# A spatial product made of seven block products, with all of v before all of u

## The reference

```
h = max(x @ w_in, 0)                      # x: 2 x 768 x 512, w_in: 512 x 1024
u, v = h[..., :512], h[..., 512:]
v_n = (v - mean(v)) / sqrt(var(v) + 1e-6) # over the 512 channels of a token
v_s = einsum('ts,bsd->btd', w_spatial, v_n) + b_spatial[None, :, None]   # w_spatial: 768 x 768
out = (u * v_s) @ w_out                   # w_out: 512 x 512
```

## Time and profile before

| | us |
|---|---|
| median of 3 runs | 501.73 |
| the profiled execution, its own time | 501.73 |
| its span (first to last instruction) | 499.9 |
| TensorE busy with matmuls | 494.2 |
| VectorE, ScalarE, GpSimd busy | 285.3, 214.9, 209.1 |

### The profile page before, as it was taken

The page is one execution under the profiler, slowest core; times in us unless marked ns, Lnnn a source line. Parts: engine busy times, 40 slices in busy tenths (PEclk is TensorE's granted clock), DMA queues, the critical chain, the costliest instruction groups (busy, mean ns, idle before and its releaser), DMA issues.

```text
span 499.9 us, 7893 instructions
## 1 busy us (share of the span) xinstructions
PE 494.2 (99%) x2822; PEld 414.2 (83%) x2822; DVE 285.3 (57%) x666; ACT 214.9 (43%) x502; POOL 209.1 (42%) x178
## 2 busy tenths in 40 slices
PE   8999999999999999999999999999999999999997
PEld 7788677887888888888888888888888998889985
DVE  5888788421379457455574654658686356521530
ACT  7988889532235533232341231324655113321121
POOL 6797576443346765762766616514330000000000
PEclk9999999999999999999999999999999999999999
DMA  8824501132223322202222022021400000110002
GB/s 235 267 89 116 182 2 44 45 126 85 84 86 101 110 84 86 82 2 85 85 85 84 1 84 74 20 88 63 147 1 1 1 1 21 43 64 0 1 24 103
DMA packets 14553, 36.29 MB, mean 73 GB/s; under 512 B 2480, under 2 KB 2480, under 8 KB 14512
## 3 DMA queue, kind: packets, MB, share of 16 engines
q1 hardware_dynamic: 12640, 32.35, 19.4%
q10 hardware_dynamic: 1872, 3.41, 1.8%
HBM read 32.61 MB, written 3.15 MB: 72 GB/s over the span
## 4 chain that ended last, share of the span: by engine, by line
PE 96%; ACT 3%; DMA 1%; issue 0%; SPq 0%; ACTq 0%
PE bank L1228 23%; PE bank L1502 15%; PE bank L1434 9%; PE bank L1359 9%; PE bank L1531 9%; PE bank L1524 9%; PE bank L1564 7%; PE bank L1284 4%; PE bank L1266 4%; PE bank L1251 3%; ACT prob L955 1%; PE bank L1298 1%; PE bank L1306 1%; DMA qk_raw<-in_qk 1%; PE bank L1331 1%; PE bank L1320 1%
## 5 line engine op out<-in xcount | busy, mean ns | idle before, releaser
L470 POOL TENSOR_TENSOR w_slot<-stage,w_slot 128x1024 fp32r<-128x1024 f32 x30 | 73.4, 2456 | 64.9 <-ACT w_slot L1025 64.8
L787 DVE TENSOR_TENSOR uT<-bank,uT 128x512 f32<-128x512 f32 x68 | 45.8, 690 | 25.1 <-PE bank L1531 23.1
L1228 PE MATMUL bank<-sp_slot,vn 128*128 128x384 f32 x288 | 50.3, 334 | 0.0
L1228 PEld LDWEIGHTS bank<-sp_slot,vn 128*128 128x128 f32 x288 | 50.0, 188 | 0.2
L955 ACT ACTIVATE prob<-prob,row_min 128x256 f32<-128x256 f32 (+1 forms) x96 | 45.9, 480 | 7.4 <-DVE row_min L605 7.4
L1502 PE MATMUL bank<-u_op,s_slot 128*128 128x512 f32 x192 | 47.6, 389 | 0.0
L1434 PE MATMUL bank<-hid,w_slot 128*128 128x512 f32 x192 | 46.9, 393 | 0.0
L1359 PE MATMUL bank<-u_split,w_slot 128*128 128x512 f32 x192 | 46.5, 391 | 0.0
L1524 PE MATMUL bank<-hid,w_slot 128*128 128x512 f32 x192 | 46.1, 389 | 0.0
L1531 PE MATMUL bank<-hid,w_slot 128*128 128x512 f32 x192 | 46.1, 389 | 0.0
L1434 PEld LDWEIGHTS bank<-hid,w_slot 128*128 128x128 f32 x192 | 35.7, 188 | 8.2 <-issue 0.9
(11 more groups left out here) (121 smaller groups left out, 837.5 us busy)
## 6 DMA issues: line engine op xcount, KB each, us to landing
stage<-in_w_ch SPq DMA_DIRECT2D x32, 512.0 KB, 3.3
qk_raw<-in_qk SPq DMA_DIRECT2D x23, 256.0 KB, 4.9
v_all<-in_v SPq DMA_DIRECT2D x12, 256.0 KB, 5.3
out_dram<-o_stage ACTq DMA_DIRECT2D x12, 256.0 KB, 2.0
stage<-in_w_spT SPq DMA_DIRECT2D x6, 384.0 KB, 3.0
stage<-in_w_in SPq DMA_DIRECT2D x4, 512.0 KB, 4.2
stage<-in_w_out SPq DMA_DIRECT2D x2, 512.0 KB, 3.6
V_raw<-in_V SPq DMA_DIRECT2D x4, 96.0 KB, 4.6
```

Source lines behind the costliest of these rows:

```text
L470: nc.gpsimd.tensor_tensor(dst[:, LO, :], stage[n % 2][:, 0:w], dst[:, HI, :].bitcast(F32), ALU.subtract).then_inc(w_lo, 1)
L787: vec.tensor_tensor(y, y_bank(e)[:], y, ALU.add).then_inc(y_sum, 1)
L1228: last = mm(out_ap, lhs(a), rhs(c), start=(n == 0), stop=(n == 3 * len(terms) - 1))
```

## The change

The spatial matrix product is cut into 2 x 2 x 2 blocks and made with 7 block products instead of 8, a Strassen-like scheme (the table `SEVEN`, which the pairs already use). The contracted tokens are halved into even and odd tiles, the output tokens into 384 and 384, the channels of two fb into 128 and 128. One group `("s", q)` stands for a batch and a pair of fb (q = 0 to 3); it makes the seven products x = 0 to 6 into four banks, each product 9 matmuls of 384 columns (3 tiles by 3 passes).

- Left operands: of each group three blocks of v (`v_one`) and four sums of blocks (`v_sum`), all split into high and low parts. Groups 0 and 1 (batch 0) do this with instructions of 384 columns, groups 2 and 3 (batch 1) with three times as many of 128 columns for the sums and for the single blocks. The four sums' low parts are four instructions of 384 columns. Group 2's low parts are made by GpSimd, the others by VectorE.
- Right operands: of the spatial weights seven blocks, four of them sums (`sum_sp`, `split_sp_sums`, on GpSimd, as is `split_sp`, the low part of the plain blocks).
- Outputs: the products are added up on VectorE (`add_bank`, `add_bias`, seven per group), with the bias of the first half of tokens; the second half gets it through `add_far` on GpSimd, which adds the difference of the two halves' biases.
- `ITEMS` is now: 12 v, 12 u, s 0, s 1, s 2, o 0 to 2, s 3, o 3 to 11. v tiles have 12 buffers of their own instead of 3.
- `LOADS` and the staging of the spatial weights: `in` 3 comes before the spatial loads, and a spatial load also waits for the sums of the pair before it. ScalarE rounds the last block of `y_split` after the spatial tiles 2 and 3, and takes no v tile before all of `y_split` is done.

The diff, cut to what the prediction speaks of:

```diff
--- before.py
+++ after.py
         LOADS = ([("w", m) for m in range(FT + 8)] + [("in", 0), ("in", 1)]
-                 + [("w", m) for m in range(FT + 8, 2 * FT)] + [("in", 2), ("sp", 0), ("sp", 5), ("in", 3)]
-                 + [("sp", s) for s in range(1, 5)] + [("out", 0), ("out", 1)])
+                 + [("w", m) for m in range(FT + 8, 2 * FT)] + [("in", 2), ("in", 3)]
+                 + [("sp", s) for s in range(NT)] + [("out", 0), ("out", 1)])
...
-        ITEMS = ([("v", 0), ("u", 0, 0), ("v", 1), ("u", 0, 1), ("v", 2), ("u", 0, 2), ("v", 3), ("u", 0, 3),
-                  ("v", 4), ("u", 1, 0), ("v", 5), ("u", 1, 1), ("u", 1, 2), ("u", 1, 3)]
-                 + [("s", 0, c, fb) for c in range(2) for fb in range(FB)]
-                 + [("v", 6), ("v", 7), ("o", 0), ("v", 8), ("o", 1), ("v", 9), ("o", 2), ("v", 10), ("o", 3),
-                    ("v", 11), ("o", 4), ("u", 2, 0), ("o", 5), ("u", 2, 1), ("u", 2, 2), ("u", 2, 3)]
-                 + [("s", 1, c, fb) for c in range(2) for fb in range(FB)] + [("o", t) for t in range(NT, TILES)])
+        ITEMS = ([("v", t) for t in range(TILES)] + [("u", c, fb) for c in range(CH) for fb in range(FB)]
+                 + [("s", 0), ("s", 1), ("s", 2), ("o", 0), ("o", 1), ("o", 2), ("s", 3)]
+                 + [("o", t) for t in range(3, TILES)])
+        V_DONE = TILES
...
+        def made(*what):
+            return sum(7 if w[0] == "s" else 1 for w in ITEMS[:item_no(*what) + 1])
+        def s_banks(q):
+            return g_ring[4:8] if q == 1 else g_ring[0:4]
+        GPART = (2, 1, 2, 3)
...
+            def add_far(q):
+                pool.wait_ge(b_diff, 1)
+                pool.wait_ge(g_dve, 7 * q + 2)
+                if q:
+                    pool.wait_ge(gate_lo, 4 * q)
+                nc.gpsimd.tensor_tensor(gpart[3][:], gpart[0][:], b_row[:, HT:S], ALU.add).then_inc(far_bias, 1)
...
+            for s in range(NT):
+                n = load_no("sp", s)
+                split_sp(s, n)
+                if s % 2:
+                    sum_sp(s // 2, n)
+                    split_sp_sums(s // 2)
+            split_v_sums(2)
+            add_far(0)
+            split_v_ones(2)
+            add_far(1)
+            split_out(load_no("out", 0))
+            split_out(load_no("out", 1))
+            add_far(2)
+            add_far(3)
...
+            def sum_v(q):
+                parts = v_blocks(q)
+                dve.wait_ge(vn_ok, NT * (q // 2 + 1))
+                if q < 2:
+                    dve.wait_ge(g_ps, made("u", q, FB - 1))
+                elif q == 2:
+                    for n in range(2):
+                        dve.wait_ge(v_one_hi[n], 3)
+                        dve.wait_ge(v_one_lo[n], 3)
+                else:
+                    dve.wait_ge(g_ps, made("s", 1))
+                def dst(name, ks):
+                    return v_sum_raw[V_BUF[q]][:, SUMS[name], ks, :]
+                for ks in parts:
+                    vec.tensor_tensor(dst("S1", ks), v_block(q, 1, 0, ks), v_block(q, 1, 1, ks),
+                                      ALU.add).then_inc(v_summed[q], 1)
+                for ks in parts:
+                    vec.tensor_tensor(dst("S3", ks), v_block(q, 0, 0, ks), v_block(q, 1, 0, ks),
+                                      ALU.subtract).then_inc(v_summed[q], 1)
+                dve.wait_ge(v_summed[q], len(parts))
+                for ks in parts:
+                    vec.tensor_tensor(dst("S2", ks), dst("S1", ks), v_block(q, 0, 0, ks),
+                                      ALU.subtract).then_inc(v_summed[q], 1)
+                dve.wait_ge(v_summed[q], 3 * len(parts))
+                for ks in parts:
+                    vec.tensor_tensor(dst("S4", ks), v_block(q, 0, 1, ks), dst("S2", ks),
...
+            def split_v_ones(q):
+                x = 0
+                for ks in v_blocks(q):
+                    for n, (r, half) in enumerate(ONES):
+                        x += 1
+                        dve.wait_ge(v_one_hi[q], x)
+                        hi, lo = v_one[V_BUF[q]][n]
+                        vec.tensor_tensor(lo[:, ks, :], v_block(q, r, half, ks), hi[:, ks, :].bitcast(F32),
+                                          ALU.subtract).then_inc(v_one_lo[q], 1)
+            def split_v_sums(q):
+                dve.wait_ge(v_sum_hi[q], 1)
+                for x in range(4):
+                    vec.tensor_tensor(v_sum[V_BUF[q]][:, LO, x, :, :], v_sum_raw[V_BUF[q]][:, x, :, :],
+                                      v_sum[V_BUF[q]][:, HI, x, :, :].bitcast(F32),
+                                      ALU.subtract).then_inc(v_sum_lo[q], 1)
...
+            def add_bank(q, dst, src, held, products, after):
+                dve.wait_ge(g_ps, made("s", q) - 7 + products)
+                if after:
+                    dve.wait_ge(g_dve, 7 * q + after)
+                vec.tensor_tensor(gpart[dst][:], gpart[src][:], s_banks(q)[held][:, 0:HT], ALU.add).then_inc(g_dve, 1)
+            def add_bias(q, dst, products):
+                dve.wait_ge(g_ps, made("s", q) - 7 + products)
+                vec.tensor_tensor(gpart[dst][:], s_banks(q)[0][:, 0:HT], b_row[:, 0:HT], ALU.add).then_inc(g_dve, 1)
+            def gate_block(q, x, after):
+                r, c = BLOCKS[x]
+                b, p = divmod(q, 2)
+                dve.wait_ge(g_dve, 7 * q + after)
+                part = gpart[GPART[x]][:]
+                vec.tensor_tensor(part, part, gate_u[2 * p + r][:, b * S + c * HT:b * S + (c + 1) * HT],
+                                  ALU.mult).then_inc(gate_ok, 1)
...
+            for t in range(TILES + 1):
+                if t < TILES:
+                    moments(t)
+                if t:
+                    normalise(t - 1)
             dve.wait_ge(b_in, 16)
-            gate_batch(0)
-            normalise_batch(1)
-            gate_batch(1)
+            vec.tensor_tensor(b_row[:, HT:S], b_row[:, HT:S], b_row[:, 0:HT], ALU.subtract).then_inc(b_diff, 1)
+            for q in range(2):
+                sum_v(q)
+                split_v_ones(q)
+                split_v_sums(q)
+            sum_v(2)
+            dve.wait_ge(g_act, by_act(item_no("s", 0)))
+            for q in range(4):
+                add_bias(q, 0, 1)
+                add_bank(q, 0, 0, 1, 2, 1)
+                add_bias(q, 2, 3)
+                gate_block(q, 0, 3)
+                dve.wait_ge(far_bias, q + 1)
+                add_bank(q, 1, 3, 2, 4, 0)
+                split_gate(q, 0)
+                add_bank(q, 1, 1, 3, 5, 4)
+                gate_block(q, 1, 5)
+                add_bank(q, 2, 0, 2, 6, 2)
+                gate_block(q, 2, 6)
+                split_gate(q, 1)
+                add_bank(q, 3, 3, 3, 7, 0)
+                gate_block(q, 3, 7)
+                split_gate(q, 2)
+                split_gate(q, 3)
+                if q == 1:
+                    sum_v(3)
+                    split_v_ones(3)
+                    split_v_sums(3)
...
+                    q = what[1]
+                    for x in range(4):
+                        round_gate(q, x)
+                    if q == 0:
+                        split_stage(load_no("out", 0))
+                        split_stage(load_no("out", 1))
+                    if q == 1:
+                        round_v_ones(3)
+                        round_v_sums(3)
...
+            def spatial(q):
+                r = V_BUF[q]
+                for x, (block, op, held, more) in enumerate(SEVEN):
+                    if x == 0:
+                        pe.wait_ge(v_one_lo[q], 3 * len(v_blocks(q)))
+                        pe.wait_ge(w_lo, load_no("sp", NT - 1) + 1)
+                    if x == 1:
+                        pe.wait_ge(v_sum_lo[q], 4)
+                        pe.wait_ge(sp_lo, 2 * TC)
+                    if x == 2:
+                        pe.wait_ge(g_dve, 7 * q + 1)
+                    if x == 5:
+                        pe.wait_ge(g_dve, 7 * q + 4)
+                    if x == 6:
+                        pe.wait_ge(g_dve, 7 * q + 5)
+                    if not more:
+                        if q < 2:
+                            pe.wait_ge(g_act, 2 * NB + 4 * q + held + 1)
+                        else:
+                            pe.wait_ge(g_dve, 7 * (0, 2)[q - 2] + (3, 2, 6, 7)[held])
+                    for j in range(TC):
+                        for n, (a, m) in enumerate(PASSES):
+                            if block in SUMS:
+                                lhs = v_sum[r][:, a, SUMS[block], j, :]
+                            else:
+                                lhs = v_one[r][ONES.index(block)][a][:, j, :]
+                            last = mm(s_banks(q)[held][:, 0:HT], lhs, sp_op[j][:, m, SP_AT[op], :],
+                                      start=not more and j == 0 and n == 0, stop=j == TC - 1 and n == 2,
+                                      skip_group_check=True)
+                    last.then_inc(g_ps, 1)
             def item(n):
```

(28 more changed lines are left out.)

268 lines of the change are left out of this document (164 added, 104 removed).

## The result

The changed kernel takes 508.23 us (median of 4, 507.01 to 509.19) against 501.75 us (4 runs, 501.67 to 501.87): a ratio of 1.0128, 95% interval 1.0104 to 1.0151. It is slower by 6.5 us, inside the range (502.0 to 508.5) and 2.5 us above the forecast of 505.7. Where the kernel before repeats within 0.2 us in these runs, the new one scatters over 2.2. Not every difference between executions is TensorE's clock: beside the experiments 6 of 37 executions of the kernel before took 504.3 to 504.5 us, 2.7 more than the others, at a mean granted clock of 1.0, and why was not looked for.

The account below looks back on a forecast made before the run. The prediction took TensorE's own work, busy 99% of the span, as the bound. From 501.73 us: -6.25 for matmuls, +0.9 small stalls, +7.2 main stall, +2.1 clock gave 505.7 us, range 502.0 to 508.5.

Parts of the forecast that it names:

- 36 matmuls, -6.25 us: Spatial product: 252 instead of 288 matmuls of 384 columns, at 0.1735 us each, saves 6.25 us.
- All v first, cost 0: v stage: VectorE ends v at about 399, before TensorE needs item 12's bank for item 20 at 402.9; cost 0.
- the 6 us for locks: v stage: 6 us assumed for VectorE and GpSimd excluding each other, on top of 31 us for 12 tiles.
- Group 0, 0.1 us: Inside group 0: waits at x = 2 for ScalarE's last u tile and x = 5 for `add_far`, 0.1 us each.
- Group 0 to 1, 0.7 us: Group 1's x = 2 waits for `add_bias` behind VectorE's leftover work: 0.15 us late, with GpSimd locks 0.7 us.
- Group 1 to 2, 7.2 us, the main term: Group 3's preparation stands ahead of group 2's `add_bias` in VectorE's list; TensorE stands 7.2 us, bounds 5.2 and 10 us.
- The clock, 2.1 us: After the long stall TensorE's first matmuls run at 1.2 instead of 2.4 GHz: 2.1 us, bounds 0 and 2.2.
- The sign, weight loads of 333 ns instead of 188: Expected in the profile for about 4 us after the stall before group 2's third product if the clock falls.
- B (clock stays): Rival: TensorE's clock stays up after the stall in group 2; 503.6 us, chance 0.26.
- C (a short preparation): Rival: group 3's preparation costs TensorE less at group 2's x = 2, so no slower; 501.6 us, chance 0.11.
- D: Rival: v tiles cost VectorE 3.16 us, not 2.56, so TensorE stands 3 us more near 403; 509 us, chance 0.08.
- E: Rival: no stall in group 2, the change does what its count says; 496.4 us, chance 0.05.

Follow-up runs that it names:

- e3: Changed kernel with ScalarE taking the square root of tile 1 ahead of the spatial weights' sums and tiles 4 and 5; 506.34 us.
- e8: e5 with VectorE reading the first bank of groups 1 and 2 ahead of the last two low parts of the group before; 495.65 us.
- e5: Changed kernel with e1 and e3 together, ScalarE's last u tile ahead of rounding group 2's sums, add_far(0) ahead of that group's low parts; 497.58 us.
- e1: Changed kernel with group 3's preparation moved behind group 2's gates on VectorE and ScalarE; 499.26 us.
- e2: Changed kernel with 36 extra matmuls into an unread bank ahead of group 2's third product; 505.74 us.
- e7: Same as e2 but with 24 extra matmuls instead of 36; 506.09 us.
- e4: Changed kernel with group 3's nine 128-column low parts made by GpSimd instead of VectorE, ahead of add_far(2); 509.92 us.

## Why the prediction was right, point by point

- **36 matmuls, -6.25 us.** Right. The products have the distance of 1.56 us, and the kernel without waits is 6.1 us of span below the one before.
- **All v first, cost 0.** Right for the banks: v and u have no idle time. Wrong in what followed. v was done at 402.2 and not 399. It began at 362.8 and not 362, and it took 39.4 us instead of 31 + 6: 2.45 of them VectorE waited for the square root of tile 1, which stood on ScalarE behind the sums and two tiles of the spatial weights, whose transfer was not done. Without that wait 37.0 are left (e3 and e8, where it is gone, take 37.6), so the 6 us for locks were about right. The prediction compared this with the bank of item 20 only. The lateness ran on through the preparation of groups 0 to 2, where VectorE had no slack, and came out at group 0's third product.
- **Group 0, 0.1 us.** This is the term that was mis-sized: 1.86 us. The prediction named both links, ScalarE's rounding and the last u tile, and put them at almost nothing, because it took v to end at 399; it also left `sum_v(2)`, 2.6 us on VectorE (413.64 to 416.27), out of the work that lies under the u items. e3 shows the part that comes from v; e5, with ScalarE's order changed as well, shows the stand gone.
- **Group 0 to 1, 0.7 us.** 0.24. Without locks the forecast had 0.15; GpSimd's nine small low parts ended at 428.21, before VectorE's last two low parts began at 428.55, so the 0.5 us of locks were not there.
- **Group 1 to 2, 7.2 us, the main term.** 7.00. From the group's end at 438.21 TensorE resumed after 10.12 us, forecast 10.3. One piece of this came right by luck: the 0.7 us of locks were expected on the last steps of the preparation, where GpSimd was idle (its output weights were done at 438.94). Instead VectorE, slowed by the same GpSimd work during group 1, read the last bank 1.08 us after the group's end and not 0.28. The preparation itself took 6.24 us (441.49 to 447.73), forecast 6.3. The 128-column additions, which no row of before showed, have the 0.20 us that the line through 32 and 224 columns gave: three in 0.69 us. e1 confirms the cause, the place in VectorE's list.
- **The clock, 2.1 us.** It fell, and cost 2.84 us. The size came from the kernel's start, where 4.6 us of work ran slowly; here it is some 6.0 us, at half the clock. The sign, weight loads of 333 ns instead of 188, is there (median 330). e2 shows the term by itself, 2.7 us of five products. The Trainium skill ("TensorE: Matmul & The Clock Gate", section "What's actually happening") says that the throttled clock is the default and that activity releases it; the windows above agree, with 0.50 while TensorE stood and the full clock again only after those 6.0 us of work.
- **The rivals.** B (clock stays) and C (a short preparation) are excluded by the windows and by the 7.00 us. D had v fall behind because a tile takes VectorE 3.16 us, and had TensorE wait near 403. A tile took 2.54 (ScalarE's square roots at 389.17, 391.71 and 394.25), and no u item waited; only the direction was D's, v later than the sum had it, and it cost 1.86 us at group 0. E's condition, `add_bias` of group 2 ahead of the preparation, is e1: 499.26 us, and not 496.4, since the stand at group 0 and its clock remain. Only e8, with the small waits out too, comes to 495.65.

Against the forecast of 505.7 that makes +1.76 at group 0's third product, -0.1 at its sixth (no wait there), -0.46 at group 1, -0.2 at group 2, +0.25 in products after waits, +0.74 of clock and +0.10 at the start: 2.1 us, or 507.8, where the profiled execution took 507.84. The median of the four is 0.4 higher; they differ by 2.2 us. The clock can be a part of that, as in e1, but not all: 507.84 and 509.19 have the same mean clock of 0.989, so that difference has another cause, which stays open.

## What to carry to other kernels

When work is cut from an engine that is busy all the time, count for each wait that the new scheme adds what stands ahead of the awaited instruction in its engine's list, not how busy that engine is on average: VectorE was busy 57% before the change, and 25 instructions in the wrong place cost more than the cut gave. A stage that finishes with slack against its own deadline must be followed to the next place where its engine has none. A TensorE that stands can pay again in clock: here 2.84 us after 6.84 us of stand, 1.7 after 2.33 in one execution, nothing after 2.65 in another. Look at each execution's mean clock before explaining a scatter by it, since some of the longer executions here have a full one.

## What the runs showed of the hardware

- After a stand of 2.33 us the clock fell when TensorE had been back at work for 1.3 us (e1, 0.50 from 421 to 424); a stand of 2.65 us left it at 1.00 in the profiled execution of e7.
- A longer stand did not cost more clock: five products took 10.65 us after 6.84 us of stand and 10.40 after 8.95 (e4).
- Filler matmuls into an unused bank held the clock in the profiled execution of e2: 36 of them, laid in a stand of 7 us, did not delay the product behind them (7.01 us late against 7.00), and the median fell by 2.5 us.
- Moving nine two-input instructions from VectorE to GpSimd lengthened VectorE's own part: three 128-column additions took 1.47 us beside GpSimd's and 0.69 alone.
